# Routing between the experts: one more round searched four bits a step, candidates made by tensor_tensor, and TensorE's search pieces moved

## The reference

```python
def _moe_ref(x, w_gate, w1, w2):
    logits = x @ w_gate                       # 3072 tokens, 8 experts
    order = np.argsort(-logits.flatten())
    ...
    for idx in order:                         # greedy: best pair of token and expert first
        tok, e = (int(idx) // E, int(idx) % E)
        if assigned[tok] >= 0 or counts[e] >= cap:
            continue
        assigned[tok] = e
        counts[e] += 1
    ...
    for e in range(E):
        h = np.maximum(x[assigned == e] @ w1[e], 0.0)
        out[assigned == e] = h @ w2[e]

def _moe2_ref(x, w_in, w_out):
    h = x @ w_in                              # 3072 x 384 by 384 x 2048
    g = h * (1.0 / (1.0 + np.exp(-h)))
    return g @ w_out
```

## Time and profile before

| | |
|---|---|
| median of 3 runs | 1082.27 us (1079.34 to 1089.83) |
| the profiled execution | 1078.51 us, of which the span is 1076.7 us |
| TensorE busy | 962.6 us (89%), mean granted clock 0.95 |
| VectorE busy | 729.9 us (68%) |
| GpSimd busy | 471.7 us (44%) |
| ScalarE busy | 412.4 us (38%) |
| DMA | 61.93 MB, 58 GB/s over the span |

### The profile page before, as it was taken

One profiled execution on the slowest core, in us unless ns is written; L12 is line 12 of the kernel. 1 busy time (PEld: TensorE's weight loads), 2 busy tenths in 40 slices (PEclk: granted clock), 3 DMA queues, 4 the chain that ended last, 5 costly groups with the idle time before them and its releaser, 6 DMA issues.

```text
span 1076.7 us, 32107 instructions
## 1 busy us (share of the span) xinstructions
PE 962.6 (89%) x13967; PEld 897.1 (83%) x13967; DVE 729.9 (68%) x1572; ACT 412.4 (38%) x930; POOL 471.7 (44%) x583
## 2 busy tenths in 40 slices
PE   4888889898888539989988999999999999999996
PEld 3777778887777429889987899899899899899996
DVE  5667676767665388887778788788788788783000
ACT  3444443444443034234334326326326326326321
POOL 3235545555550024345434445535535535535532
PEclk9999998999997559999998999999999999999998
DMA  8322222111110030030040030030030030030000
GB/s 294 124 70 59 66 52 59 48 48 48 47 49 18 9 139 1 1 139 23 1 140 16 9 125 23 15 126 23 15 120 28 16 118 23 23 117 23 23 1 22
DMA packets 31563, 61.93 MB, mean 58 GB/s; under 512 B 3776, under 2 KB 23360, under 8 KB 31040
## 3 DMA queue, kind: packets, MB, share of 16 engines
q1 hardware_dynamic: 28352, 50.45, 14.5%
q0 software_dynamic: 3072, 9.44, 2.7%
HBM read 50.44 MB, written 9.44 MB: 56 GB/s over the span
## 4 chain that ended last, share of the span: by engine, by line
PE 49%; DVE 14%; issue 1%; POOL 1%; DMA 1%; ACT 0%; DVEq 0%
PE PS L1272 47%; DVE above L1075 3%; DVE cand L1104 3%; DVE cs L1079 2%; DVE w_lo L1218 2%; PE PS L1235 1%; DVE delta L1086 1%; DMA xg<-x_rows,idx 1%; PE PS L1259 1%; PE PS L1290 1%; DVE weighed L1083 0%; DVE over L1120 0%; POOL xg L959 0%; PE PS L1250 0%; DVE w_lo L1214 0%
## 5 line engine op out<-in xcount | busy, mean ns | idle before, releaser
L952 POOL TENSOR_TENSOR act_t<-whole,act_t 128x384 fp32r<-128x384 f32 x192 | 210.6, 1100 | 303.7 <-ACT whole L1010 302.9
L1004 ACT ACTIVATE act_t<-PS 128x384 fp32r<-128x384 f32 x192 | 94.6, 492 | 376.4 <-PE PS L1272 376.4
L1272 PE MATMUL PS<-w_out_hi,act_t 128*128 128x384 f32 x768 | 222.7, 346 | 1.6 <-POOL act_t L952 1.6
L1272 PE MATMUL PS<-x2T,w_in_hi 128*128 128x384 f32 x768 | 223.3, 345 | 0.1
L1272 PEld LDWEIGHTS PS<-x2T,w_in_hi 128*128 128x128 f32 x768 | 142.2, 191 | 3.5 <-POOL x2T L952 2.0
L1272 PEld LDWEIGHTS PS<-w_out_hi,act_t 128*128 128x128 f32 x768 | 142.2, 190 | 1.9 <-POOL act_t L952 1.9
L1272 PE MATMUL PS<-w_out_lo,act_t 128*128 128x384 f32 x384 | 133.0, 346 | 0.0
L1272 PE MATMUL PS<-x2T,w_in_lo 128*128 128x384 f32 x384 | 132.0, 344 | 0.0
L1272 PE MATMUL PS<-xgT,w_hi 128*128 128x384 f32 x384 | 110.1, 346 | 0.6 <-ACT whole L1008 0.6
L1272 PE MATMUL PS<-act_t,w_hi 128*128 128x384 f32 x384 | 106.4, 337 | 0.0
L1075 DVE TENSOR_TENSOR above<-V,cand 128x576 bf16<-128x576 f32 x112 | 91.7, 818 | 3.9
(11 more groups left out here) (204 smaller groups left out, 1848.6 us busy)
## 6 DMA issues: line engine op xcount, KB each, us to landing
w_sb<-moe_w SPq DMA_DIRECT2D x16, 1536.0 KB, 8.2
k_in<-k_t SPq DMA_DIRECT2D x24, 192.0 KB, 4.2
KQ<-q_t SPq DMA_DIRECT2D x48, 96.0 KB, 2.2
v_in<-v_t SPq DMA_DIRECT2D x24, 192.0 KB, 3.1
x_rows<-ysb SPq DMA_DIRECT2D x48, 96.0 KB, 2.2
w_in<-moe_w_in SPq DMA_DIRECT2D x1, 3072.0 KB, 11.8
w_out<-moe_w_out SPq DMA_DIRECT2D x1, 3072.0 KB, 20.1
xg<-x_rows,idx POOLq DMA_INDIRECT x24, 3.1
```

The source lines that it names most:

```text
L952: nc.gpsimd.tensor_tensor(lo, whole_of(t), hi.bitcast(F32), ALU.subtract).then_inc(rest_ok, 1)
L1004: nc.scalar.activation(hi, src, func).then_inc(hi_ok, 1)
L1272: ins = mm(o, a, b, start=start, stop=stop, skip_group_check=True)
```

## The change

Round 1 is searched four bits a step as round 0 is, so that `digits` is cut into `tally` and `share`, which `search` issues among the passes. The new candidates are made by a `tensor_tensor` from the threshold after that has been updated, where one `tensor_scalar` with two scalar operands made them from the old threshold and the new bits. The table of the pieces is new: round 1 has one of its own (`AT_D`), the later rounds all stand 36 passes ahead of their turn, and the spread over the first counts is 5 passes longer.

```diff
+BY_DIGITS = 2
@@ search_pairs
                     if i < PARTS:
                         split_w2(r - 1, i)
                     weigh(i + 1, r, i, delta[:, :])
+                    chain(v.tensor_tensor(cur[:, :], cur[:, :], delta[:, :], ALU.bitwise_xor))
                     if i + 1 < PAIRS:
-                        v.tensor_scalar(cand[:, :], pair_i[:, i + 1, :], cur[:, 0:1], delta[:, 0:1], ALU.bitwise_xor,
-                                        ALU.bitwise_xor).then_inc(dv, 1)
-                        chained["n"] += 1
-                    chain(v.tensor_tensor(cur[:, :], cur[:, :], delta[:, :], ALU.bitwise_xor))
+                        chain(v.tensor_tensor(cand[:, :], pair_i[:, i + 1, :], cur[:, 0:1].to_broadcast([C, 3]), ALU.bitwise_xor))
@@ search_digits
+                    if r and i < PARTS:
+                        split_w2(r - 1, i)
-                    dve.wait_ge(over_ps, i + 1)
+                    dve.wait_ge(over_ps, DIGITS * r + i + 1)
...
-                        v.tensor_scalar(cand16[:, :], digit_i[:, i + 1, :], cur[:, 0:1], delta[:, 0:1], ALU.bitwise_xor,
-                                        ALU.bitwise_xor).then_inc(dv, 1)
-                        chained["n"] += 1
                         chain(v.tensor_tensor(cur[:, :], cur[:, :], delta[:, :], ALU.bitwise_xor))
+                        chain(v.tensor_tensor(cand16[:, :], digit_i[:, i + 1, :], cur[:, 0:1].to_broadcast([C, CANDS]), ALU.bitwise_xor))
@@ route
-                if start:
-                    search_digits()
+                if r < BY_DIGITS:
+                    for q in range(PARTS if r else 0):
+                        split_w1(r - 1, q)
+                    search_digits(r)
@@ search
+                if r < BY_DIGITS:
+                    if i >= 2 * DIGITS:
+                        place(r, i - 2 * DIGITS)
+                    elif i % 2 == 0:
+                        tally(r, i // 2)
+                    else:
+                        share(r, i // 2)
@@ the pieces
-            AT = [17 * i + 5 * min(i, PARTS) for i in range(COUNTS)]
-            AT += [AT[-1] + 21] + [AT[-1] + 45 + 6 * h for h in range(NT // HOT)]
-            AHEAD = [0, 4, -6] + [-48] * (E - 3)
-            pieces = [(PASSES * (r - 1) + at + AHEAD[r], r, i) for r in range(1, E) for i, at in enumerate(AT)]
+            AT = [17 * i + 5 * min(i, PARTS + 1) for i in range(COUNTS)]
+            AT_D = [10 + 22 * (i // 2) + 6 * (i % 2) + 4 * min(i // 2, PARTS) for i in range(2 * DIGITS)]
+            def with_places(at):
+                return at + [at[-1] + 21] + [at[-1] + 45 + 6 * h for h in range(NT // HOT)]
+            AHEAD = -36
+            pieces = [(at, 1, i) for i, at in enumerate(with_places(AT_D))]
+            pieces += [(PASSES * (r - 1) + at + AHEAD, r, i) for r in range(BY_DIGITS, E) for i, at in enumerate(with_places(AT))]
```

More of the change, by code:

```diff
@@ L1081, in weigh @@
             def weigh(i, r, w, o):
-                dve.wait_ge(cnt_ps, COUNTS * (r - 1) + i + 1)
+                dve.wait_ge(cnt_ps, COUNTS * (r - BY_DIGITS) + i + 1)
                 chain(v.scalar_tensor_tensor(weighed[:, :, :].rearrange("p c e -> p (c e)"), PS[:, 3, 0:3 * E], CAP - 0.5,
@@ L1102, in search_pairs, with search_digits @@
                     weigh(i + 1, r, i, delta[:, :])
+                    chain(v.tensor_tensor(cur[:, :], cur[:, :], delta[:, :], ALU.bitwise_xor))
                     if i + 1 < PAIRS:
[L1104 to L1107 removed]
+                        chain(v.tensor_tensor(cand[:, :], pair_i[:, i + 1, :], cur[:, 0:1].to_broadcast([C, 3]), ALU.bitwise_xor))
                 count(1, COUNTS - 1, r)
[L1109 removed]
+                dve.wait_ge(cnt_ps, COUNTS * (r - BY_DIGITS) + COUNTS)
                 chain(v.tensor_scalar(full[:, :], PS[:, 3, 0:E], CAP - 0.5, None, ALU.is_ge))
[L1112 removed]
+            def search_digits(r):
                 chain(v.tensor_scalar(cand16[:, 0:CANDS // 2], digit_i[:, 0, 0:CANDS // 2], -1, None, ALU.bitwise_xor))
@@ L1122, in search_digits @@
                                     ALU.is_ge).then_inc(over_ok, 1)
-                    dve.wait_ge(over_ps, i + 1)
+                    if r and i < PARTS:
+                        split_w2(r - 1, i)
+                    dve.wait_ge(over_ps, DIGITS * r + i + 1)
                     v.tensor_scalar(hits[0:nc_, :], PS[0:nc_, 3, 0:E], CAP - 0.5, 1.0 if i == 0 else float(1 << (28 - 4 * i)),
                                     ALU.is_ge, ALU.mult).then_inc(hits_ok, 1)
-                    dve.wait_ge(hits_ps, i + 1)
+                    dve.wait_ge(hits_ps, DIGITS * r + i + 1)
                     if last:
@@ L1142, in search_digits @@
                     else:
-                        v.tensor_scalar(cand16[:, :], digit_i[:, i + 1, :], cur[:, 0:1], delta[:, 0:1], ALU.bitwise_xor,
-                                        ALU.bitwise_xor).then_inc(dv, 1)
-                        chained["n"] += 1
                         chain(v.tensor_tensor(cur[:, :], cur[:, :], delta[:, :], ALU.bitwise_xor))
+                        chain(v.tensor_tensor(cand16[:, :], digit_i[:, i + 1, :], cur[:, 0:1].to_broadcast([C, CANDS]), ALU.bitwise_xor))
             def route(r):
-                start = r == 0
                 ebc = lambda t: t.unsqueeze(2).to_broadcast([C, NT, E])
@@ L1231, in search @@
             def search(r, i):
-                if i < COUNTS:
-                    pe.wait_ge(cs_ok, COUNTS * (r - 1) + i + 1)
+                if r < BY_DIGITS:
[5 more added lines that the diff above has]
+                        share(r, i // 2)
+                elif i < COUNTS:
+                    pe.wait_ge(cs_ok, COUNTS * (r - BY_DIGITS) + i + 1)
                     mm(PS[:, 3, 0:3 * E], ones_b[:, :], cs[:, :, :].rearrange("p c e -> p (c e)"), start=True, stop=True).then_inc(cnt_ps, 1)
@@ L1252, in place, with tally, share @@
                     last.then_inc(hot_used, 1)
-            def digits():
-                for i in range(DIGITS):
-                    c0 = 0 if i == DIGITS - 1 else 1
-                    pe.wait_ge(over_ok, i + 1)
-                    for m in range(NT):
-                        last = mm(PS[0:CANDS - c0, 3, 0:E], over[:, m, c0:CANDS], onehot[:, m, :], start=(m == 0), stop=(m == NT - 1))
-                    last.then_inc(over_ps, 1)
-                    pe.wait_ge(hits_ok, i + 1)
-                    mm(PS[:, 4, 0:E], ones_b[0:CANDS - c0, :], hits[0:CANDS - c0, :], start=True, stop=True).then_inc(hits_ps, 1)
-            PLACES = 1 + NT // HOT
-            AT = [17 * i + 5 * min(i, PARTS) for i in range(COUNTS)]
-            AT += [AT[-1] + 21] + [AT[-1] + 45 + 6 * h for h in range(NT // HOT)]
-            AHEAD = [0, 4, -6] + [-48] * (E - 3)
-            pieces = [(PASSES * (r - 1) + at + AHEAD[r], r, i) for r in range(1, E) for i, at in enumerate(AT)]
+            def tally(r, i):
+                c0 = 0 if i == DIGITS - 1 else 1
+                pe.wait_ge(over_ok, DIGITS * r + i + 1)
+                for m in range(NT):
+                    last = mm(PS[0:CANDS - c0, 3, 0:E], over[:, m, c0:CANDS], onehot[:, m, :], start=(m == 0), stop=(m == NT - 1))
+                last.then_inc(over_ps, 1)
+            def share(r, i):
+                c0 = 0 if i == DIGITS - 1 else 1
+                pe.wait_ge(hits_ok, DIGITS * r + i + 1)
+                mm(PS[:, 4, 0:E], ones_b[0:CANDS - c0, :], hits[0:CANDS - c0, :], start=True, stop=True).then_inc(hits_ps, 1)
+            PLACES = 1 + NT // HOT
+            AT = [17 * i + 5 * min(i, PARTS + 1) for i in range(COUNTS)]
[5 more added lines that the diff above has]
+            pieces += [(PASSES * (r - 1) + at + AHEAD, r, i) for r in range(BY_DIGITS, E) for i, at in enumerate(with_places(AT))]
             passes = [0]
@@ L1385, in turn @@
                             fourth(k, j, h, 1)
-            digits()
+            for i in range(DIGITS):
+                tally(0, i)
+                share(0, i)
             for i in range(PLACES):
```

2 lines of the change are left out of this document (removed).

## The result

The change made the kernel slower: 1101.16 us (median of 4 runs, 1095.85 to 1102.78) against 1080.8 (4 runs, 1078.69 to 1089.83), a ratio of 1.0156 with an interval of 1.012 to 1.0191. The forecast was 1068, the range 1062 to 1074. The profiled execution took 1100.44 us, with a span of 1098.7.

The account below looks back on a forecast made before the run. TensorE's passes, waits and inserted work were taken to bound the routed part. Turn 1 -11.4, steady gains in turns 1 to 6 -3.6, turn 0 +2.5: together -12.5 us from 1080.8 to 1068, range 1062 to 1074.

Parts of the forecast that it names:

- turn 1: Round 2's late place in turn 1: moved to where the other rounds stand, 93.0 falls to 81.6, 11.4 us off.
- The wait of 6.49 us: End of turn 1: TensorE waits for the sums of round 3's first count; forecast to go with round 2's new place.
- that chain: VectorE's preparation from last hot to next first count's sums; held to end behind split_w1 at fixed passes, leaving 2.1 us.
- The 14 us of turn 1: VectorE's time before the change for round 3's preparation, with only 35 passes (6.1 us) between last hot and pass 384.
- A wait for a first count in turn 1: Sign of a wrong prediction: turn 1 still waiting for the sums of a first count.
- Turns 2 to 6: Steady turns: sixth-count wait goes (0.88 us), one more late wait (0.3 us); net 0.6 us off each turn.
- The 22 passes for the sixth count: Steady turns: sixth count gets 22 passes behind the fifth instead of 17, 0.88 us, about all of its 0.82 us wait.
- VectorE stays late: Rival, turns 1 to 6: 0.9 us of waiting stays, 0.3 comes per turn; -5.3 us, 1075.5 us; chance 0.22.
- The late gathers: Rival, turns 1 to 6: GpSimd held 4 us more, so 2 us wait and 1.7 clock each; +9.7, 1090.5; chance 0.04.
- Candidates: nothing: Search steps: two-operand candidates keep two operations of about 0.2 us; 0.3 us at most either way over round 0's loop.
- Turn 0: +2.5 forecast: Four-bit search: tallies and shares +6.6, counts -2.1, late search waits -1.2, shorter gather wait -0.8 us.
- the first rival: End of turn 0: the clock holds behind the gather wait, another 1.7 us off; -14.2 us, 1066.5 us; chance 0.25.

## Why the prediction was wrong

**What bounds the kernel, and turn 1: the right wait, the wrong length.** The wait of 6.49 us went, and with it the 1.56 us one. The step that failed is "most of that chain does not start from the hot: it ends behind the four `split_w1`", from which followed that "those sums stay due near pass 384, and a count at pass 396 has 12 passes, 2.1 us, in hand". For the steady turns of before that reading was right: `split_w1` waited for ScalarE there, 1.84 + 0.93 = 2.8 us:

```profile
647.98 1.83 DVE L1214 TENSOR_TENSOR w_lo<-w_sb,w_hi 128x768 fp32r<-128x768 f32 x2 [1.84 <-ACT w_hi L1015]
...
650.73 2.03 DVE L1214 TENSOR_TENSOR w_lo<-w_sb,w_hi 128x768 fp32r<-128x768 f32 x2 [0.93 <-ACT w_hi L1015]
```

In the change it waits for nothing (655.78 above), since VectorE comes to it too late. The chain then hangs on `idx` alone, and it is not of one length: 12.5 us in the steady turns of before, 11.1 us with the gathers a step later, 13.1 us with two rests overdue, 15.4 us with three. Between before and the change VectorE's own part grew from 9.7 to 15.4 us, 4.3 of it in the three held operations. The forecast took that part to be fixed. The 14 us of turn 1, in which `idx` was late before too, stood in the same paragraph and should have been the row to take for a later `idx`. It would have given a wait of 14 - 12.6 = 1.4 us and a sign to doubt the forecast. Turn 1 gained 6.1 us, not 12.0 (11.4 and the steady 0.6). A wait for a first count in turn 1 was named as a sign that the prediction is wrong, and it came.

**Turns 2 to 6: 5 x -0.6 = -3.0 forecast, +19.3 measured.** The same step failed here: 2.93 us of wait in each of turns 1 to 5, a fallen clock behind it in some, and beside that smaller waits for counts (in all 23 waits with 21.9 us, of which five make 14.6; six of 0.66 at pass 159 are the form's). The 22 passes for the sixth count did what was said: with AHEAD -48 and the same spread no wait is left there, and a turn falls from 81.7 to 80.97 us in the new form and to 80.7 in the old, where 81.0 was forecast. That edit's mechanism was right, and its size near enough.

**The rivals.** "VectorE stays late" was the right one, with 0.22. It named stalls beside GpSimd, but priced them at 0.9 + 0.3 us a turn from operations of the search, not from the preparation. Slower by over 1%, as measured, had been given 0.06. The late gathers did not come: there was indeed slack there, and GpSimd's 3.83 us were spent before the gathers, not behind them.

**Candidates: nothing.** Wrong in size: 0.28 to 0.69 us a turn. The count of operations was right, but not which operation meets which rest: in the old form `above` began 0.17 us earlier and was through before the next rest, in the new one it was held.

The rule weighed there (the Trainium skill, SBUF — State Buffer, section "Who interferes with whom") says that a tensor_tensor contends only with a GpSimd instruction that reads SBUF. I had set it aside for the row at 472.34. The runs mostly bear it out: beside an indirect DMA alone such an operation took 0.36 us (at 642.67 with AHEAD -48, at 650.31 with later gathers). It took 1.83 only where a rest was already due behind the gather, and it ended 0.2 us after that rest. So I had read the row at 472.34 wrongly: it too ends, at 474.16, 0.2 us after a rest that follows the gather,

```profile
472.91 1.03 POOL L952 TENSOR_TENSOR act_t<-whole,act_t 128x384 fp32r<-128x384 f32 x1
```

and it is the rest that held it. The measurement adds to the rule: by itself the operation at 648.84 would have been through 0.2 us before the recorded start of the rest at 649.41, and it was held all the same. GpSimd's recorded spans are rough, so whether the hold begins before the rest does is not shown.

**Turn 0: +2.5 forecast, +3.2 measured.** The terms were off in ways that partly cancel; that the sum lies near is luck. A tally costs 0.88 us (0.69 forecast) and a share 0.31 (0.13), so the eight steps cost 9.5 us, not 6.6. The wait for the gather at the end was 2.21 us, as forecast, but the clock stayed full behind it, as the first rival had it: 1.7 us back. With these two the sum is +3.7. The low clock at the start of turn 0, which was to stay as it is, ended 4.0 us behind the first pass in this execution and 5.0 behind it before, worth 0.5 us; it ended 8.6 behind it when the change was profiled again, and turn 0 took 93.9 us there. The +3.2 is worth no more than to about 2 us.

**The range** held neither the backlog nor the form. The bound for VectorE was taken from rows of the search, and no end of the range was worked out from the preparation with all its held operations (three by 1.4, 4.3 us), though such holds stand in the trace of before: the 1.82 us at 472.34 lies beside a gather that had waited 3.84 us for `idx`, the same picture.

## What to carry to other kernels

When a producer is moved later, look at which engine waits for it with work behind that falls due meanwhile: once released, that engine runs its backlog in one block. An engine whose operations it holds up, as GpSimd does VectorE's here, is stretched over the whole block if it starts from the same event. A slack read from one steady turn is not a constant: take the longest duration that the same chain shows anywhere in the trace, with the circumstances that made it so, and only then spend the slack. And an operation more between a held one and a costly one can be worth several times its own duration, when the costly one just slipped in ahead of the next hold.

## What the runs showed of the hardware that was not expected

Whether a VectorE operation is held depends on what is due behind GpSimd's DMA instruction, as told above: 0.36 us with the rest not yet due, 1.83 us with it due, for the same shapes and the same gather of 0.99 us. The margin is small: with AHEAD -48 the operation began at 642.67, and ScalarE's copy, which makes the rest due, ended at 642.79.

A group of tiny matmuls among 384-column passes costs a fixed 0.28 us and 0.025 us a matmul (24 of 15 columns of weights and 8 columns of data).

A wait of 2.21 us at 489.66 was followed by a full clock, while one of 1.95 us before, with one of 1.06 us close ahead of it, was followed by 0.66. The 2.93 us waits were followed by low clock in some turns and not in others of the same execution. The length of one wait alone does not say whether the clock falls.

The last matmul of the attention, which is the same code in all kernels, started between 359.7 and 378.3 us in 14 profiles, at 364.8 in that of the change. The window over it in the kernel before, in the form of the earlier trace rows:

```profile
0.00:360.00 360.00, 301.35 (x9912) 272.40 (x9912) 231.65 (x454) 146.18 (x343) 154.21 (x295) 0.94 0.26 74
```

and in the kernel with old form and uniform gathers, the longest one:

```profile
0.00:378.00 378.00, 313.58 (x9910) 283.35 (x9910) 231.88 (x454) 146.30 (x343) 153.96 (x295) 0.89 0.25 71
```

VectorE, ScalarE and GpSimd are busy for the same time within 0.3 us, and TensorE has the same matmuls (two more or fewer at the window's edge); its granted clock is 0.94 in the one and 0.89 in the other. Why the clock falls more often in some executions was not tried. It is why kernels were compared here by the routed part as well as by their times.
